# MoE scores interleaved with the last projections, and the rows of u in six buffers summed inside the MoE steps

## The reference, cut to what matters

```python
# attention: B, H, S, D = 2, 8, 768, 64; block 32, window 16
k_sum = k.reshape(B, H, nb, 32, D).max(axis=3)
v_sum = v.reshape(B, H, nb, 32, D).mean(axis=3)
a = softmax(concat([mask(scale * q @ k.T), scale * q @ k_sum.T + log(32)]))
x = a @ concat([v, v_sum])                      # regrouped to (B, S, 512)
# experts: 4 experts, the best 2 by gate
logits = x @ w_gate; w = softmax over the two best logits
for e in range(4):
    q, k, v = x @ wq[e], x @ wk[e], x @ wv[e]   # 64 wide
    y = softmax(causal(scale * q @ k.T)) @ v @ wo[e]
    x2 += w[e where chosen] * y
# MLP
h = relu(x2.T @ w_tok1) @ w_tok2
u = x2 + h.T
out = u + relu(u @ w_ch1) @ w_ch2
```

## Time and profile before

| what | value |
|---|---|
| median of 3 runs | 495.92 us (492.92 to 496.09) |
| the profiled execution, its own time | 492.22 us |
| its span in the profile | 490.2 us |
| PE busy | 449.2 us, 92% of the span |
| DVE, ACT, POOL busy | 250.6, 193.2, 28.8 us |
| chain that ended last: PE, DVE, ACT, DMA, issue | 75%, 13%, 4%, 2%, 4% |

### The profile page before, as it was taken

How to read it: one execution, slowest core, us unless ns; L and a number is a source line. 1 busy time by engine, 2 the same in 40 slices (tenths; PEclk the granted TensorE clock), 3 DMA queues, 4 the chain that set the end, 5 groups by cost and what they waited for, 6 DMA issues and landing times.

```text
span 490.2 us, 8342 instructions
## 1 busy us (share of the span) xinstructions
PE 449.2 (92%) x3250; PEld 381.7 (78%) x3250; DVE 250.6 (51%) x512; ACT 193.2 (39%) x578; POOL 28.8 (6%) x36
## 2 busy tenths in 40 slices
PE   7677996998986889969989999999999999999997
PEld 3456995786764569957867899889988999889985
DVE  6897368776558982678884565311212121112201
ACT  5956445754326874467771244201211021002200
POOL 3056800000000000000000000000000000000000
PEclk9999997999998999979999999999999999999999
DMA  8684540000582054000003650014001300020001
GB/s 286 196 208 134 169 186 0 1 2 1 139 248 80 4 178 166 1 0 1 3 0 96 227 193 1 0 44 150 2 0 44 119 31 0 21 79 29 1 23 43
DMA packets 19268, 38.09 MB, mean 78 GB/s; under 512 B 2112, under 2 KB 7328, under 8 KB 19232
## 3 DMA queue, kind: packets, MB, share of 16 engines
q1 hardware_dynamic: 17504, 34.45, 21.9%
q10 hardware_dynamic: 1728, 3.15, 1.7%
HBM read 30.42 MB, written 6.29 MB: 75 GB/s over the span
## 4 chain that ended last, share of the span: by engine, by line
PE 75%; DVE 13%; issue 4%; ACT 4%; DMA 2%; SPq 1%; ACTq 0%; POOL 0%; DVEq 0%; POOLq 0%
PE ps_s L500 38%; PE ps_t L500 22%; PE ps_o L500 6%; PE ps_x L500 4%; PE ps_t L660 4%; DVE nmaxA L1076 2%; DVE KL L1115 2%; DVE PTA L1094 1%; DMA u_rows<-US 1%; DMA VT<-in_vT 1%; DVE XT_l L1101 1%; DVE US L1240 1%; ACT PA L857 1%; DVE vsum L1227 1%; DVE nmaxM L1167 1%
## 5 line engine op out<-in xcount | busy, mean ns | idle before, releaser
L500 PE MATMUL ps_s<-UT_h,ch_h 128*128 128x384 f32 x192 | 65.0, 339 | 0.1
L500 PE MATMUL ps_s<-UT_h,ch_l 128*128 128x384 f32 x192 | 65.0, 339 | 0.0
L500 PE MATMUL ps_s<-UT_l,ch_h 128*128 128x384 f32 x192 | 64.9, 338 | 0.0
L1055 ACT ACTIVATE HID_h<-ps_s 128x384 fp32r<-128x384 f32 x48 | 23.6, 492 | 93.8 <-PE ps_s L500 93.7
L1372 DVE SCALAR_TENSOR_TENSOR HID_l<-ps_s,HID_h 128x384 fp32r<-128x384 f32 x48 | 26.8, 558 | 65.9 <-ACT HID_h L1055 65.9
L500 PE MATMUL ps_t<-ch_h,HID_h 128*128 128x512 f32 x144 | 56.7, 394 | 0.0
L500 PE MATMUL ps_t<-ch_h,HID_l 128*128 128x512 f32 x144 | 56.2, 391 | 0.0
L500 PE MATMUL ps_t<-ch_l,HID_h 128*128 128x512 f32 x144 | 56.1, 390 | 0.0
L1380 DVE TENSOR_TENSOR OS<-ps_t,UR 128x512 f32<-128x512 f32 x12 | 8.3, 692 | 83.6 <-PE ps_t L500 83.6
L857 ACT ACTIVATE PA<-ps_s,nmaxA 128x120 f32<-128x120 f32 x96 | 33.3, 367 | 16.5 <-DVE nmaxA L1076 16.5
L500 PEld LDWEIGHTS ps_s<-UT_h,ch_h 128*128 128x128 f32 x192 | 36.1, 188 | 0.6 <-DVE UT_l L1245 0.5
(11 more groups left out here) (197 smaller groups left out, 909.4 us busy)
## 6 DMA issues: line engine op xcount, KB each, us to landing
VW<-in_vw SPq DMA_DIRECT2D x12, 384.0 KB, 7.8
KP<-in_kT SPq DMA_DIRECT2D x8, 384.0 KB, 6.8
VT<-in_vT SPq DMA_DIRECT2D x8, 384.0 KB, 5.9
u_rows<-US ACTq DMA_DIRECT2D x12, 256.0 KB, 2.1
ch_raw<-in_ch SPq DMA_DIRECT2D x4, 768.0 KB, 6.5
US<-u_rows SPq DMA_DIRECT2D x4, 768.0 KB, 5.7
ch_raw<-in_ch SPq DMA_DIRECT2D x12, 256.0 KB, 5.0
UR<-u_rows SPq DMA_DIRECT2D x4, 768.0 KB, 4.6
```

Of the source, the lines that this page charges most:

```text
L500: return pe.matmul(out, lhsT, rhs, start=start, stop=stop)
L1055: act.activation(HID_h[:, m, :], bank[m % 4][:, 0:GS], ACT.Relu).then_inc(g_hh, 1)
```

## The change

Eight things are altered; no arithmetic is.

1. PE: scores of MoE units 0 and 1 are put behind projections 5 and 6. ACT: exponentials 0 and 1 are put ahead of the high parts of projections 6 and 7. DVE: maxima 0 and 1 are put ahead of the low parts of projections 6 and 7, with three gate steps behind maxima 1 and three behind the last low part. The loops begin at k = 2.
2. US1 becomes six buffers. Three take the place of the old ones; three, and PTM2, lie in the second half of KW (window keys of pairs 2 and 3); SPREAD lies in an unused part of `raw`. `sum_x2` moves into the MoE steps (end of step k where k - 2 is in `TURN_AT`), tile 5 into the token MLP; `st_u` becomes six semaphores.
3. New waits for the stores of tiles 0 to 2: in batch 1 ahead of the window keys of pair 2 (ACT and DVE), and in the channel MLP ahead of the seventh `HID_h` (ACT).
4. ACT: `m_out_hi` goes ahead of the exponentials of its step.
5. ACT: the exponentials of attention unit 2 go behind `a_to_sbuf` of unit 0, in both batches.
6. DVE, batch 0: the value sums of pair 1 go behind `a_to_sbuf` of unit 0.
7. SP: `load_first_queries(0, 1)` goes ahead of `place_means(0, 0)`.
8. PE: 13 warm-up matmuls instead of 16.

```diff
@@ constants, buffers
-N_WARM = 16
+N_WARM = 13
-        US1 = sb("US1", [P, NUS, DM], F32)
+        US1 = [None] * TQ
+        for t in range(NUS, TQ):
+            US1[t] = sb(f"US1_{t}", [P, DM], F32)
+        wide, SPREAD = raw[:, :, 0:E * HD], raw[:, :, E * HD:2 * E * HD]
+        PTM[2], spare = at("PTM2", [P, 1024], F32, windows_at + PAIRS // 2 * NW * KC * 4)
+        for t in range(NUS):
+            US1[t], spare = at(f"US1_{t}", [P, DM], F32, spare)
@@ SP
             load_keys(0, 3)
+            load_first_queries(0, 1)
             place_means(0, 0)
             load_windows(0, 0, 2)
-            load_first_queries(0, 1)
@@ PE
+                pe.wait_ge(c_pool, N_CONST)
                 for g in range(4, 8):
                     m_project(b, g)
-                pe.wait_ge(c_pool, N_CONST)
-                for k in range(MU + 3):
+                    if 5 <= g < 7:
+                        m_scores(b, g - 5)
+                for k in range(2, MU + 3):
@@ ACT
+                if b > 0 and q == 1 and i == 0:
+                    for j in range(NUS):
+                        act.wait_ge(st_u[j], b * 16)
...
-                    if 3 <= k < NU:
+                    if k < NU:
                         a_exps(b, k)
...
-                for g in range(4, 7):
-                    m_project_hi(b, g)
+                m_project_hi(b, 4)
+                m_project_hi(b, 5)
                 act.wait_ge(m_g, b * NGATE + 3)
                 act.activation(gate_e[:, :, :], gate_x[:, :, :], ACT.Exp).then_inc(m_ge, 1)
+                m_exps(b, 0)
+                m_project_hi(b, 6)
+                m_exps(b, 1)
                 m_project_hi(b, 7)
-                for k in range(MU + 3):
+                for k in range(2, MU + 3):
...
+                    if k in TURN_AT:
+                        m_out_hi(b, TURN_AT.index(k))
                     if k < MU:
                         m_exps(b, k)
                     if k - 1 in TURN_AT:
                         m_x2(b, TURN_AT.index(k - 1))
-                    if k in TURN_AT:
-                        m_out_hi(b, TURN_AT.index(k))
...
-                    if more and t + 1 in SCORES_BEFORE:
+                    if more and t + 1 in SCORES_BEFORE[:2]:
                         a_exps(b + 1, SCORES_BEFORE.index(t + 1))
...
+                    if first and m == KCH // 2:
+                        for t in range(NUS):
+                            act.wait_ge(st_u[t], 16 * B)
@@ DVE
+                if b > 0 and pairs[0] == PAIRS // 2:
+                    for t in range(NUS):
+                        dve.wait_ge(st_u[t], b * 16)
...
+                    if b == 0 and k == 2:
+                        value_sums(0, (1,))
...
                 m_project_lo(b, 5)
                 advance(gate_steps, 2)
+                m_maxima(b, 0)
                 m_project_lo(b, 6)
+                m_maxima(b, 1)
+                advance(gate_steps, 3)
                 m_project_lo(b, 7)
-                for k in range(MU + 3):
+                advance(gate_steps, 3)
+                for k in range(2, MU + 3):
...
-                    if k < 2:
-                        advance(gate_steps, 3)
...
+                    if k - 2 in TURN_AT:
+                        sum_x2(b, TURN_AT.index(k - 2))
...
-                for t in range(NUS):
-                    dve.wait_ge(m_xl, b * TQ + (t + 1))
-                    sum_x2(b, t)
...
-                    if 2 <= t < 2 + TQ - NUS:
-                        sum_x2(b, t - 2 + NUS)
+                    if t == 2:
+                        sum_x2(b, TQ - 1)
```

More of the change, by code:

```diff
@@ L143, in program @@
         gate_s = sb("gate_s", [P, 2, TQ], F32)
-        us1_at = place[0]
-        US1 = sb("US1", [P, NUS, DM], F32)
+        US1 = [None] * TQ
+        for t in range(NUS, TQ):
+            US1[t] = sb(f"US1_{t}", [P, DM], F32)
         region1 = place[0]
-        wide = raw[:, :, 0:E * HD]
+        wide, SPREAD = raw[:, :, 0:E * HD], raw[:, :, E * HD:2 * E * HD]
         QT = sb("QT", [P, PAIRS, S], F32)
@@ L186, in program @@
             PTM[i], p = at(f"PTM{i}", [P, 1024], F32, p)
-        PTM[2], spread_at = at("PTM2", [P, 1024], F32, us1_at)
-        SPREAD, end_spread = at("SPREAD", [P, 2, E * HD], F32, spread_at)
-        assert end_spread <= region1
         region5 = max(p, endA)
+        PTM[2], spare = at("PTM2", [P, 1024], F32, windows_at + PAIRS // 2 * NW * KC * 4)
+        for t in range(NUS):
+            US1[t], spare = at(f"US1_{t}", [P, DM], F32, spare)
+        assert spare <= region2
         QS, endM = at("QS", [P, E, S], F32R, region5)
@@ L287, in program @@
         m_t2 = sem("m_t2"); m_u = sem("m_u")
-        st_u = [sem(f"st_u{i}") for i in range(NUS)]
+        st_u = [sem(f"st_u{t}") for t in range(TQ)]
         g_us = sem("g_us"); g_ur = sem("g_ur")
@@ L398, in _ @@
                 sp.dma_start(ch1_raw[:, k, :], ch1_d[k * P:(k + 1) * P, :]).then_inc(ld_c1, 16)
-            for i in range(NUS):
-                sp.wait_ge(st_u[i], 16 * (1 + TQ // NUS))
+            for t in range(GT):
+                sp.wait_ge(st_u[t], 16)
             load_u(0, US, g_us)
@@ L404, in _ @@
                 sp.dma_start(ch2_raw[:, k, :], ch2_d[k * P:(k + 1) * P, :]).then_inc(ld_c2[k // 4], 16)
-            for i in range(NUS):
-                sp.wait_ge(st_u[i], 16 * (1 + B * TQ // NUS))
+            for t in range(TQ):
+                sp.wait_ge(st_u[t], 16 * B)
             load_u(0, UR, g_ur)
@@ L936, in m_spread @@
                 act.wait_ge(m_d, b * TQ + (t + 1))
-                if t == 0:
-                    act.wait_ge(st_u[2], b * (16 * TQ // NUS) + 16)
                 if t >= 2:
@@ L952, in m_x2 @@
                 act.activation(X2_h[:, t, :], ps_x[:, :], ACT.Copy).then_inc(m_xh, 1)
-            for i in range(NUS):
-                act.sem_inc(st_u[i], 16)
             def store_u(b, t):
                 act.wait_ge(m_u, b * TQ + (t + 1))
-                act.dma_start(u_d[bass.ds(b * S + t * P, P), :], US1[:, t % NUS, :]).then_inc(st_u[t % NUS], 16)
+                act.dma_start(u_d[bass.ds(b * S + t * P, P), :], US1[t][:, :]).then_inc(st_u[t], 16)
             def c_u_hi(g, j):
@@ L1044, in _ @@
                 key_windows(0, 0, i)
-            for k in range(3):
+            for k in range(2):
                 a_exps(0, k)
@@ L1177, in m_to_sbuf @@
                     dve.wait_ge(m_av, b * NVG + (GROUP_OF[u - 3] + 1))
-                if u == 2:
-                    for i in range(2):
-                        dve.wait_ge(st_u[i], b * (16 * TQ // NUS) + 16)
                 dve.tensor_copy(PTM[u % 3][:, 0:width], ps_t[:, 0, 0:width]).then_inc(m_pt0, 1)
@@ L1230, in sum_x2 @@
             def sum_x2(b, t):
-                dve.wait_ge(st_u[t % NUS], b * (16 * TQ // NUS) + (16 * (t // NUS) + 16))
-                dve.tensor_tensor(US1[:, t % NUS, :], X2_h[:, t, :].bitcast(F32), X2_l[:, t, :].bitcast(F32),
+                dve.wait_ge(m_xl, b * TQ + (t + 1))
+                if b > 0:
+                    dve.wait_ge(st_u[t], b * 16)
+                dve.tensor_tensor(US1[t][:, :], X2_h[:, t, :].bitcast(F32), X2_l[:, t, :].bitcast(F32),
                                   ALU.add).then_inc(m_xn, 1)
@@ L1239, in add_tokens @@
                 dve.wait_ge(m_xn, b * TQ + (t + 1))
-                dve.tensor_tensor(US1[:, t % NUS, :], token_bank[b][t % 2], US1[:, t % NUS, :], ALU.add).then_inc(m_u, 1)
+                dve.tensor_tensor(US1[t][:, :], token_bank[b][t % 2], US1[t][:, :], ALU.add).then_inc(m_u, 1)
             def c_u_lo(g, j):
@@ L1361, in _ @@
             a_maxima(0, 2)
-            value_sums(0, (1,))
             a_maxima(0, None, 1)
```

## The result

Median 499.51 us (499.45 to 501.26, 6 runs) against 495.36 (492.27 to 496.22, 6 runs) for the kernel before: ratio 1.0108 [1.0072, 1.0144]. The forecast was 500.7 us in a range of 495.5 to 505.5. The profiled execution of after took 501.26 us (span 499.2, mean granted clock 0.956); the one of before 492.22 (span 490.2, 0.979). Their spans differ by 9.0 us, the medians by 4.2: each profile caught one end of its kernel's spread. So the profiles show where the time goes, and the medians how much it is. Of the other five executions of after, four had spans of 497.3 to 497.4 at a clock of 0.966, and one 499.0 at 0.959. In all that follows, ratios leave out runs more than 1.5% above the fastest of their kernel, while medians and ranges take them in.

A forecast was written before the change was run, and what follows sets the result against it. PE, busy 449.2 of 490.2 us, was taken as the bound. Terms of +12.2 (MoE start), -4.8 (passage), -1.0 (start) and -1.6 (output high parts) make +4.8 on a 495.92 us median: 500.7 us, range 495.5 to 505.5.

The forecast's parts named there:

- What bounds the kernel: Whole kernel: PE, busy 449.2 of 490.2 us; time lost ahead of the filled MoE steps is not caught up.
- Part 1, the chain: MoE start: ACT and DVE alternate, links sum to 17.3 us, transpositions of unit 1 come 4.5 us later per batch.
- Part 1, the clock: After PE's second gap at the MoE start: low clock for 4.4 us again, costing 1.6 a batch, between nothing and 2.2.
- Part 2 and part 5, the passage: From batch 0 to 1: store wait and sums removed, exponentials 2 moved, clock stays high; -4.8 us, between -2 and -6.
- part 5's 0.4: Passage between batches: the PTA copy fills time ahead of exponentials 2 on ACT, so values 0 come 0.4 us earlier.
- price nothing: MoE steps of batch 0: DVE's five moved sums of 0.6 us each fit into its gaps, at no cost.
- Parts 6 to 8, the start: Kernel start: shorter warm-up, earlier query load and moved value sums give -1.0 us, between -2.5 and +0.5.
- Part 4: End of MoE steps: output high part ready earlier, -1.3 us in batch 0 and -0.3 in batch 1; between 0 and -3.
- The sum: Whole kernel: all terms together +4.8 us, giving a median of 500.7 us.
- no low clock at the second return: MoE start: clock stays high or soon recovers after PE's second gap; +1.6 us in all, 497.5 us; chance 22%.
- the gap simply goes: MoE start: ACT and DVE still overlap, saving 4.38 us twice; 479.7 us in all; chance 6%.
- The third rival: Passage gives back only -2 us, or two MoE-start gaps keep the clock low for 7 us: +7.6, 503.5 us; chance 22%.

The follow-up runs named there:

- first two experiments: Changed kernel with the early scores, maxima and exponentials order undone: 486.75 us, ratio 0.9896; kernel before with that order alone added: 506.44 us, ratio 1.0274.
- third: Changed kernel with ACT's high part of keys 6 ahead of exponentials 0, that of keys 7 ahead of exponentials 1: 489.71 us.
- fourth: Changed kernel with 19 idle matmuls ahead of the scores of unit 3 and 22 behind them: 495.16 us, ratio 1.0048 to the kernel before.
- ninth: The third experiment's kernel with 10 idle matmuls ahead of the scores of unit 3 and 12 behind: 485.69 us, ratio 0.9821 to the kernel before.
- fifth experiment: Kernel before with only the six buffers, sums in the MoE steps and new store waits added: 492.18 us, ratio 0.9938.
- seventh: The first experiment's kernel with 16 warm-up matmuls, value sums and query load at their old places: 487.37 us, ratio 0.9845 to the kernel before.
- eighth: The first experiment's kernel with only the warm-up matmuls put back to 16: 486.08 us, ratio 0.9834 to the kernel before.
- sixth experiment: The first experiment's kernel with output high parts put back behind the exponentials: 490.75 us, ratio 0.9938 to the kernel before.
- first experiment: Changed kernel with drains again ahead of scores, maxima and exponentials 0 and 1, all else kept: 486.75 us, ratio 0.9896 to the kernel before.
- tenth experiment: The third experiment's kernel with DVE's maxima 2 and PTM copy ahead of low part 7, and 10 idle matmuls only ahead of scores 3: 486.09 us.
- eleventh: The tenth experiment's kernel without the idle matmuls: 487.05 us, ratio 0.9851 to the kernel before.

## Why the prediction came out as it did

**What bounds the kernel.** Right. PE's longest waits are still those ahead of transpositions 1, and what was lost there was not caught up: transpositions 1 of batch 0 are 6.0 us later than before (84.85 to 90.81), values 1 behind the low clock 8.8 (88.88 to 97.68), and the last transpositions ahead of the output projection of pair 4 are 9.1 late (117.27 to 126.39). Only at that projection, where part 4 acts, does it fall to 7.5 (120.05 to 127.54).

**Part 1, the chain.** Right in mechanism and nearly in size: the sum of links gave 17.3 us from maxima 0 to transpositions 1, the trace has 16.94. With that the term is +4.2 a batch instead of +4.5. The first two experiments show that this part alone makes both gaps, and the third that ACT's order makes them.

**Part 1, the clock.** The mis-sized term: "I take 1.6", with 2.2 as the upper bound, because "it stays low for 4.4 us again". In the profiled execution it stayed low for 6.2 us behind the second return (5.6 in batch 1), and from transpositions 1 to values 1 it took 6.87 us instead of 4.03 (6.58 instead of 4.01): +2.8 and +2.6, together 5.4, outside the bounds. The step that fell short is that the stretch would last as long as the one before. The fourth and ninth experiments, which remove the low clock alone, give back 3 to 5 us for both batches together, 1.5 to 2.5 a batch; so the medians leave room for 1.6, at the low end of what they show. The Trainium skill ("TensorE: Matmul & The Clock Gate", section "Terms") would put an estimated 3.1 us on a stretch of 6.2 and 2.8 on one of 5.6, half of each; the trace has 2.8 and 2.6. PE has no wait in these stretches, and where the small rest goes is not shown.

**Part 2 and part 5, the passage.** Forecast -4.8, found -5.3: 4.3 up to values 0 of batch 1 (19.52 to 15.20), and 1.0 behind it, where the clock no longer falls (25.92 to 24.94 us from values 0 to the value projection; forecast 0.6). DVE has no wait for `u_rows` left. Of its terms, part 5's 0.4 was 0.2 at most. The new waits for stores cost nothing to be seen, as stated. But "price nothing" for the sums in the MoE steps was too low: in the profiled executions the lag grows by 0.3 us there in batch 0 and by 1.1 in batch 1 (238.92 to 264.35), and by 0.6 and 1.2 where part 2 stands alone (fifth experiment). For batch 1 the forecast charged about 1.0, for these sums and a weight splitting together, under part 4.

**Parts 6 to 8, the start.** Forecast -1.0; the profiled execution was 1.7 later there, outside the +0.5 of the bounds. The wait for queries went as stated, but the gain did not reach the end of the start: the clock was low in this execution at 12 to 19 (a mean of 0.53), 30 to 36 and 46 to 49, where it was full in that of before. The seventh and eighth experiments show no gain from these parts. What I left out is how much the clock of this stretch differs from execution to execution: the eight profiled kernels that share the changed start reach the 25th matmul of the value projection between 48.3 and 53.1 us, the four with the old start between 49.6 and 53.2. That is more than the edit is worth. Whether 13 warm-up matmuls also bring low stretches oftener than 16 is not shown.

**Part 4.** Forecast -1.3 and -0.3. On the traces PE's wait shrank from 1.93 to 0.30 us in batch 0, and all of it arrived: the lag goes from 9.1 to 7.5 there. In batch 1 it shrank from 1.93 to 0.91, and the lag goes from 10.1 to 9.1. With what the sums cost in the MoE steps, which the part 2 paragraph had feared for batch 1, the net is -1.3 and about +0.1, close to the forecast. The sixth experiment puts the part at 2.1 to 4.0 us, more than the -1.6: the gap that it closes can bring the clock down too. The sixth experiment's own profile has that at 256 us, for 1.6 us, and the fifth's at 261. But it is not there each time: the kernel before has the same wait of 1.93 us at 256.99 and full clock behind it. How often it comes, and so its share of the medians, is not shown.

**The sum.** Terms of the profiled execution: 1.7 + 2 x 4.2 + 5.4 - 1.3 - 5.3 + 0.1 = +9.0, and the spans differ by 9.0. Forecast +4.8; medians +4.2, ratio +5.3 us. The forecast of the median was right in its sign, its main mechanism and its sum. That it came so close is partly luck, for smaller errors cancel: by the experiments part 1 costs 10.5 to 13.5 us (forecast 12.2), part 2 gains 2.9 to 3.1 with its price in the MoE steps (forecast 4.8 with part 5, before what it charged under part 4), part 4 gains 2.1 to 4.0 (1.6), and the start gains nothing that shows (1.0). The two profiles differ more than the medians because the one of before was short and the one of after long, 1.7 us of it at the start. The rival "no low clock at the second return" is refuted by the stretches; "the gap simply goes" is refuted by the waits. The third rival's "two gaps keep the clock low for 7 us" is close to what the profiled execution shows (6.2), though its time is not that of the median, and its smaller gain at the passage is not what the trace has.

## What to carry to other kernels

Before work is moved ahead in a stream, write the new streams of the two engines side by side and add the links: where engine A's next instruction waits for B's last and B's next for A's, the two do not overlap any more, however early the inputs are. Here the scores could come early without lengthening the chain (third experiment), as long as the high part of the next keys stood on ACT ahead of the exponentials. They gained nothing either: no kernel with early scores is clear of the first experiment's, which has the old order. And where a chain leaves PE with gaps of about 2 us among sparse work, ask what the clock does behind them: some ten idle matmuls ahead of the work and as many behind it cost nothing that shows, and gave back 4 us of 490. Filling one of two such gaps (tenth experiment) did not keep the clock.

## What the runs showed of the hardware

The granted clock fell to 0.50 not only in gaps of 4.4 us (2.0 us into the gap before, 4.3 us into the first one after), but 1.8 us into a gap of 2.38 (third experiment, 82.8 us). It also fell after gaps had ended, with PE at work again: 1.6 us after one of 2.39 (eleventh, 212.8), 1.4 us after one of 1.97 (tenth, 85.5), and 1.2 us after one of 1.76 (fifth and sixth, at 260.3 and 255.7). Yet behind 1.93 us at 256.99 in the kernel before, and behind 1.76 at 120.54 in the sixth, it stayed at 1.00. So the length of a gap alone does not decide it in these runs.

How long it stayed low with PE filled again was not fixed either: 4.4 us before, 5.5 in the third experiment (87.55 to about 93), 6.2 and 5.6 in the changed kernel.

And executions of kernels with the same start differ there by stretches at the low clock: after's profiled execution has them at 12 to 19, 30 to 36 and 46 to 49 us, the first experiment's at 25 to 35 (0.70 and 0.61 as means of five) and none at 12 to 19 or 45 to 50. Runs of one kernel spread over about 1%, and the longer ones have the lower mean clock (fourth experiment: 1.000 at 493.5 us, 0.979 at 498.8). That the start makes this difference is likely, but not shown for other runs than the profiled ones.
